# First y tiles written straight into x, products dealt anew over the chunks, and one reciprocal in place of the forward scans

## The reference, cut to what matters

```python
for t in range(S):                       # attention, per batch b and head h
    cur = einsum('bhd,bhe->bhde', u * kt, vt)
    y[:, :, t] = einsum('bhd,bhde->bhe', rt, state + cur)
    state = wt[..., None] * state + einsum('bhd,bhe->bhde', kt, vt)
h = gelu(x @ w_in); u, v = split(h)
v_s = einsum('ts,bsd->btd', w_sg, norm(v) * g_ln) + b_sg
x = x + (u * v_s) @ w_out
u = x + token_mlp(x);  out = u + relu(u @ w_ch1) @ w_ch2
```

## Time and profile before

| what | value |
|---|---|
| median of 3 runs | 410.09 us (410.06 to 410.10) |
| profiled execution | 410.41 us, its span 408.9 us |
| granted TensorE clock, mean | 0.995 |
| busy in the span | TensorE 397.7 us, VectorE 196.7, GpSimd 167.6, ScalarE 109.7 |

### The profile page before, as it was taken

How to read it: one execution, slowest core, us unless ns; L and a number is a source line. 1 busy time by engine, 2 the same in 40 slices (tenths; PEclk the granted TensorE clock), 3 DMA queues, 4 the chain that set the end, 5 groups by cost and what they waited for, 6 DMA issues and landing times.

```text
span 408.9 us, 6916 instructions
## 1 busy us (share of the span) xinstructions
PE 397.7 (97%) x2682; PEld 384.9 (94%) x2682; DVE 196.7 (48%) x402; ACT 109.7 (27%) x218; POOL 167.6 (41%) x186
## 2 busy tenths in 40 slices
PE   6899899999999999999999999999999999999997
PEld 6789788899989999899999999999999999999996
DVE  5688989777977344323442756351132123103301
ACT  3465233464531020475001202340031013002300
POOL 6658659665765355386799990000000000000000
PEclk9999899999999999999999999999999999999999
DMA  9999555473541002002112410000100100000001
GB/s 151 233 202 187 99 117 105 101 145 79 98 135 40 0 2 78 2 1 79 23 55 77 132 63 2 0 2 19 40 0 2 38 21 1 10 31 21 0 21 38
DMA packets 60130, 25.04 MB, mean 61 GB/s; under 512 B 51136, under 2 KB 58176, under 8 KB 60096
## 3 DMA queue, kind: packets, MB, share of 16 engines
q1 hardware_dynamic: 60096, 24.58, 27.0%
HBM read 22.22 MB, written 2.36 MB: 60 GB/s over the span
## 4 chain that ended last, share of the span: by engine, by line
PE 89%; DVE 7%; issue 2%; ACT 1%; DVEq 0%; ACTq 0%
PE bank L1037 24%; PE bank L1039 24%; PE bank L1038 24%; PE bank L1127 4%; PE bank L1051 3%; PE bank L1220 2%; PE bank L1123 2%; PE bank L1160 2%; PE bank L1088 2%; DVE pre L831 1%; DVE suf L822 1%; PE bank L1106 1%; DVE am L855 1%; DVE x L885 1%; PE bank L1178 1%
## 5 line engine op out<-in xcount | busy, mean ns | idle before, releaser
L744 ACT ACTIVATE ha_hi<-bank 128x384 fp32r<-128x384 f32 x48 | 23.6, 492 | 113.1 <-PE bank L1039 113.1
L963 DVE SCALAR_TENSOR_TENSOR ha_lo<-bank,ha_hi 128x384 fp32r<-128x384 f32 x48 | 26.8, 558 | 50.2 <-ACT ha_hi L744 50.2
L1037 PE MATMUL bank<-c_hi,ha_lo 128*128 128x384 f32 x144 | 48.2, 335 | 0.0
L1039 PE MATMUL bank<-c_hi,ha_hi 128*128 128x384 f32 x144 | 48.1, 334 | 0.0
L1039 PE MATMUL bank<-u2T_hi,c_hi 128*128 128x384 f32 x144 | 48.1, 334 | 0.0
L1038 PE MATMUL bank<-c_lo,ha_hi 128*128 128x384 f32 x144 | 48.1, 334 | 0.0
L1037 PE MATMUL bank<-u2T_hi,c_lo 128*128 128x384 f32 x144 | 48.1, 334 | 0.0
L1038 PE MATMUL bank<-u2T_lo,c_hi 128*128 128x384 f32 x144 | 48.1, 334 | 0.0
L968 DVE TENSOR_TENSOR x<-bank,x 128x384 f32<-128x384 f32 x12 | 6.7, 558 | 65.3 <-PE bank L1039 65.3
L1037 PE MATMUL bank<-sg_hi,z_lo 128*128 128x384 f32 x96 | 32.5, 339 | 0.4 <-DVE sg_lo L935 0.4
L1039 PE MATMUL bank<-sg_hi,z_hi 128*128 128x384 f32 x96 | 32.1, 334 | 0.0
(11 more groups left out here) (146 smaller groups left out, 910.7 us busy)
## 6 DMA issues: line engine op xcount, KB each, us to landing
raw<-in_moe_w_ch SPq DMA_DIRECT2D x12, 384.0 KB, 3.1
kc<-in_k SPq DMA_DIRECT2D x12, 192.0 KB, 4.4
rc<-in_r SPq DMA_DIRECT2D x12, 192.0 KB, 4.8
vn<-in_v SPq DMA_DIRECT2D x12, 192.0 KB, 4.4
raw<-in_moe_w_sg SPq DMA_DIRECT2D x6, 384.0 KB, 3.3
out<-x SPq DMA_DIRECT2D x12, 192.0 KB, 1.9
raw<-in_moe_w_in SPq DMA_DIRECT2D x4, 384.0 KB, 4.9
raw<-in_moe_w_tok SPq DMA_DIRECT2D x4, 384.0 KB, 3.3
```

Source lines behind the costliest of these rows:

```text
L744: sc.activation(ha[0][:, i, :], bank[:, 0:HALF], ACT.Relu).then_inc(act_out, 1)
L963: ve.scalar_tensor_tensor(ha[1][:, i, :], bank[:, 0:HALF], 0.0, ha[0][:, i, :].bitcast(F32), ALU.max, ALU.subtract).then_inc(dve_out, 1)
L1037: te.matmul(dst, left[1], right[0], start=first, stop=False)
L1039: return te.matmul(dst, left[0], right[0], start=False, stop=last)
```

## The change

- `decays`: the four forward scans and the 112x4 reciprocal are replaced by one reciprocal of the whole `suf` (112x512), into `pre`. `pre_done` counts 1 per chunk, the semaphore `inverted` is gone, and `turn_w` waits for the suffix scans instead of `pre`.
- `YR` is 5: `y_tile` of chunks 0 to 4 writes straight into x; `x_tile` is left for chunks 5 to 11. The general path overwrites these tiles after waiting for `y_done`. The preset of x leaves out the five tiles. `yt` has three buffers in turn (`BR`), for the diagonal term only.
- `SLOT` begins with chunk 5 in place of 4, the products are dealt anew, and one "sg" product more is in `TAIL`. The w_in splits come one chunk later.
- The ten range checks are in order and spread over chunks 1 to 3; `mark_range`, `sum_range` and `count_range` are in chunk 4.
- SP: v and r before ub, the check tile and k, r, v of later chunks in another order, w one chunk later.
- Filler: 14 matmuls in place of 32, none after chunk 1.

```diff
-YR = 4
+YR = 5
+BR = 3
 SLOT = {
-    (4, 0): [("xT", 0, 0), ("xT", 0, 1)], (4, 2): [("v", 0, 0)],
-    (5, 0): [("v", 0, 1), ("xT", 0, 2)], (5, 1): [("xT", 0, 3)], (5, 2): [("u", 0, 0)],
...
+    (5, 0): [("xT", 0, 0), ("xT", 0, 1)], (5, 1): [("v", 0, 0), ("xT", 0, 2)], (5, 2): [("xT", 0, 3)],
+    (6, 0): [("v", 0, 1), ("xT", 0, 4)], (6, 1): [("v", 0, 2), ("wsg", 0, 0)], (6, 2): [("u", 0, 0), ("wsg", 0, 1)],
+    (7, 0): [("v", 0, 3), ("xT", 0, 5)], (7, 1): [("v", 0, 4), ("wsg", 0, 2)], (7, 2): [("u", 0, 2), ("wsg", 0, 3)],
+    (8, 0): [("v", 0, 5)], (8, 1): [("wsg", 0, 4), ("u", 0, 4), ("wsg", 0, 5)], (8, 2): [("u", 0, 6), ("wsg", 0, 6)],
+    (9, 0): [("wsg", 0, 7), ("u", 0, 1)], (9, 1): [("wsg", 0, 8), ("u", 0, 3), ("wsg", 0, 9)],
+    (9, 2): [("u", 0, 5), ("wsg", 0, 10)],
+    (10, 0): [("wsg", 0, 11), ("u", 0, 7)], (10, 1): [("sg", 0, 0)], (10, 2): [("sg", 0, 1)],
+    (11, 0): [("sg", 0, 2)], (11, 1): [("sg", 0, 3)],
 }
...
                 if n:
                     dve.wait_ge(rp_done, n)
-                ve.reciprocal(pre[0:QP, :, 0:1], suf[0:QP, :, 0:1]).then_inc(inverted, 1)
-                dve.wait_ge(inverted, n + 1)
-                for p in range(NP):
-                    src = bw[0:QP, PART * p:PART * p + PART - 1]
-                    ve.tensor_tensor_scan(pre[0:QP, p, 1:PART], src, ones[0:QP, 1:PART], pre[0:QP, p, 0:1], ALU.mult, ALU.bypass
-                                          ).then_inc(pre_done, 1)
+                ve.reciprocal(pre[0:QP, :, :], suf[0:QP, :, 0:PART]).then_inc(pre_done, 1)
...
-                dst = y_place(n) if n < YR else by[:, 0:C]
-                ve.tensor_tensor(dst, by[:, 0:C], y_place(n), ALU.add).then_inc(y_done, 1)
+                dst = x[:, 0, n, :] if n < YR else by[:, 0:C]
+                ve.tensor_tensor(dst, by[:, 0:C], yt[:, n % BR, :], ALU.add).then_inc(y_done, 1)
...
                 if n == YR - 1:
-                    count_range()
+                    mark_range()
...
                 if n == YR - 1:
-                    bound_x()
-                    x_tile(0)
-                    x_tile(1)
-                if n == YR:
-                    x_tile(2)
-                    x_tile(3)
+                    count_range()
                 y_tile(n)
...
                 if n:
-                    pe.wait_ge(pre_done, NP * n)
+                    pe.wait_ge(suf_done, NP * n)
                 turn(bw, w_tile(n)).then_inc(wt_done, 1)
...
-            keep_busy(4)
+            keep_busy(2)
             turn_w(0)
             turn_k(0)
             turn_r(0)
-            keep_busy(8)
+            keep_busy(2)
             turn_w(1)
+            keep_busy(2)
...
-                if n < YR:
+                if n < 2:
                     keep_busy(2)
                 outputs(n)
...
-                if n < YR:
-                    keep_busy(3)
+                if n < 2:
+                    keep_busy(2)
```

More of the change, by code:

```diff
@@ L60 @@
 SLOT = {
[6 rows of a table removed]
-    (9, 0): [("wsg", 0, 8), ("u", 0, 5)], (9, 1): [("wsg", 0, 9), ("u", 0, 7)], (9, 2): [("wsg", 0, 10), ("wsg", 0, 11)],
-    (10, 0): [("sg", 0, 0)], (10, 1): [("sg", 0, 1)], (10, 2): [("sg", 0, 2)],
-    (11, 0): [("sg", 0, 3)], (11, 1): [("sg", 0, 4)],
[4 rows of a table added]
+    (9, 0): [("wsg", 0, 7), ("u", 0, 1)], (9, 1): [("wsg", 0, 8), ("u", 0, 3), ("wsg", 0, 9)],
[3 rows of a table added]
 }
-TAIL = ([("sg", 0, i) for i in range(5, 8)] + [("xT", 1, i) for i in range(6)] + [("out", 0, i) for i in range(6)]
+TAIL = ([("sg", 0, i) for i in range(4, 8)] + [("xT", 1, i) for i in range(6)] + [("out", 0, i) for i in range(6)]
         + [("v", 1, i) for i in range(6)] + [("u", 1, i) for i in range(8)] + [("sg", 1, i) for i in range(8)]
@@ L175, in build @@
     rku = put("rku", [PART, H, D])
-    yt = put("yt", [PART, YR - 1, C])
+    yt = put("yt", [PART, BR, C])
     ub = put("ub", [PART, C])
@@ L379, in _ @@
             load_k(1)
+            load_r(1)
+            load_v(0)
             sp.dma_start(ub[:, :], u.rearrange("(a h) d -> a (h d)", a=1).to_broadcast([PART, C])).then_inc(ub_in, 16)
-            load_v(0)
-            load_r(1)
             load_w(2)
@@ L394, in _ @@
             load_v(2)
+            load_w(4)
+            load_w(5)
+            sp.dma_start(check_w[:, :].rearrange("p (h x) -> p h x", h=H),
+                         w[1].rearrange("h (p j) d -> p h (j d)", j=PJ)).then_inc(check_in, 16)
+            load_k(4)
+            load_r(4)
+            load_v(3)
             load_raw(0)
             load_raw(1)
-            later = {2: [2], 3: [3, 4], 4: [5], 5: [6], 6: [7], 7: [8], 8: [9, 10], 9: [11], 10: [12], 11: [13, 14]}
-            for n in range(2, NCH):
+            later = {3: [2], 4: [3], 5: [4], 6: [5], 7: [6], 8: [7, 8], 9: [9, 10], 10: [11, 12], 11: [13, 14]}
+            for n in range(3, NCH):
                 if n + 2 < NCH:
@@ L403, in _ @@
                     load_v(n + 1)
-                if NC <= n + 4 < NCH:
-                    load_w(n + 4)
+                if NC <= n + 3 < NCH:
+                    load_w(n + 3)
                 for i in later.get(n, []):
@@ L475, in general_path @@
                 gp.tensor_tensor(gd[:, 1:2], gu[:, 0:1], gu[:, 0:1], ALU.add)
+            pool.wait_ge(y_done, YR)
             for b in range(B):
@@ L502, in _ @@
             for b in range(B):
-                gp.memset(x[:, b, :, :].rearrange("p c n -> p (c n)"), -BIG).then_inc(preset, 1)
+                c = 0 if b else YR
+                gp.memset(x[:, b, c:NC, :].rearrange("p c n -> p (c n)"), -BIG).then_inc(preset, 1)
             gp.memset(wn[:, :, :, D:HP].rearrange("p a h d -> p (a h) d"), 1.0).then_inc(preset, 1)
@@ L509, in split_high @@
                 if name in ("tok1", "tok2"):
-                    pool.wait_ge(x_out, NCH)
+                    pool.wait_ge(x_out, NCH - YR)
                 elif name == "ch1" and i < 4:
@@ L545, in scale_r @@
                 pool.wait_ge(rt_copied, n + 1)
-                pool.wait_ge(pre_done, NP * (n + 1))
+                pool.wait_ge(pre_done, n + 1)
                 if n >= 2:
@@ L554, in diagonal_v @@
                 pool.wait_ge(dg_done, n + 1)
-                if n >= YR:
-                    pool.wait_ge(x_out, n - YR + 2)
-                gp.tensor_tensor(y_place(n).rearrange("p (h d) -> p h d", h=H),
+                if n >= BR:
+                    pool.wait_ge(y_done, n - BR + 1)
+                gp.tensor_tensor(yt[:, n % BR, :].rearrange("p (h d) -> p h d", h=H),
                                  vn[:, n % VR, :].rearrange("p (h d) -> p h d", h=H),
@@ L600, in chunk, with high_part, chunk_end, low_parts @@
                     diagonal_products(n + 1)
-            def chunk_end(n):
+            def high_part(n):
                 if n in early:
                     split_high(*early[n])
+            def chunk_end(n):
+                high_part(n)
                 if n + 1 < NCH:
                     scale_r(n + 1)
+                low_parts(n)
+            def low_parts(n):
                 if n in early:
@@ L619, in rest @@
                 gp.tensor_copy(flag[:, :], nhalf[:, :]).then_inc(flagged, 1)
-                chunk_end(YR - 1)
+                low_parts(YR - 1)
                 for n in range(YR, NCH):
@@ L623, in rest @@
                     chunk_end(n)
-                for i in range(5, 8):
+                for i in range(4, 8):
                     split_gated(0, i)
@@ L649, in _ @@
             chunk(YR - 1)
+            high_part(YR - 1)
+            scale_r(YR)
             pool.wait_ge(ok_counted, 1)
@@ L689, in check_range @@
                 if i:
-                    act.wait_ge(checked, CHECK_ORDER.index(i))
+                    act.wait_ge(checked, i)
                 if i < NC:
@@ L713, in take_job @@
                     elif b and i == 0:
-                        act.wait_ge(x_out, NCH)
+                        act.wait_ge(x_out, NCH - YR)
                     dst = (xT if kind == "xT" else u2T)[b][0]
@@ L774, in _ @@
             check_range(1)
-            checks = {0: (2, 3), 1: (6, 7, 8), 2: (9, 4, 5)}
+            checks = {1: (2, 3), 2: (4, 5, 6), 3: (7, 8, 9)}
             for n in range(NCH):
@@ L883, in x_tile @@
                 dst = x[:, n // NC, n % NC, :]
-                src = y_place(n) if n < YR else by[:, 0:C]
-                ve.scalar_tensor_tensor(dst, src, okm[:, 1:2], dst, ALU.min, ALU.max).then_inc(x_out, 1)
+                ve.scalar_tensor_tensor(dst, by[:, 0:C], okm[:, 1:2], dst, ALU.min, ALU.max).then_inc(x_out, 1)
             def mark_range():
@@ L1011, in _ @@
                     diagonal(n + 1)
+                if n == YR - 1:
+                    bound_x()
                 for b, i in v_jobs(n):
@@ L1113, in outputs @@
                 if n > YR:
-                    pe.wait_ge(x_out, n)
+                    pe.wait_ge(x_out, n - YR)
                 elif n:
@@ L1146, in free_bank @@
                 else:
-                    pe.wait_ge(x_out, NCH)
```

(13 more changed lines are left out.)

21 lines of the change are left out of this document (4 added, 17 removed), and 4 rows, old and new, of the table SLOT.

## The result

| | before | after |
|---|---|---|
| median of 4 runs | 410.10 us (410.06 to 413.89) | 422.82 us (419.94 to 424.51) |
| profiled execution | 410.41 us, span 408.9 | 422.69 us, span 421.2 |
| granted clock, mean | 0.995 | 0.976 |

The change makes the kernel slower, by a ratio of 1.029 (95% interval 1.026 to 1.033). The forecast was 419.6 us.

What follows compares the result with a forecast made beforehand. It took TensorE as the bound, with time won or lost only in chunks 0 to 5. Terms 3.4 + 2.8 + 3.3 gave 9.5 us more: 419.9 us profiled, 419.6 as median; range 410.5 to 431.

Steps and rivals of the forecast that it cites:

- The likeliest case: Whole kernel: the long reciprocal holds up the early chunks, 9.5 us more, 419.6 us; chance 62%.
- The reciprocal is paid per element: VectorE's 112x512 reciprocal: the 24 ns left over recur with every element, 7.0 ns each, so 3.75 us is taken.
- The period 5.3 + R: Chunks 1 to 4: mask to mask takes 5.3 us plus the reciprocal's time R, 9.05 us at full clock.
- The half-way value of the clock: Chunks 1 to 4: period 9.8 us, between full clock and 10.5 at half clock; 39.0 us in place of 36.2.
- Chunk 0 keeps its 6.2 us: Chunk 0 has no decays of its own in its period, so it stays at 6.2 us, from 16.75 to 22.95.
- First mask of chunk 5: Start and chunks 0 to 4: this mask comes at 62.35 us in place of 58.91, 3.4 us later.
- Work not yet done at that mask: Products that stood in chunk 4 now come after chunk 5's first mask: 2.8 us of TensorE work.
- From chunk 5, 3.3 us: Chunk 5 on: TensorE idles 2.2 us in chunk 5, 1.0 in chunk 9, 0.8 elsewhere, less 0.7 idle now.
- three slow x tiles: Chunk 3 before: takes 10.4 us since three x tiles in SBUF take 1.84 us in the mean, not 0.62.
- a reciprocal of 0.7 us: First rival, pipelined reciprocal: first mask 12.3, chunk 5's mask at 46.2, 9.9 us less, 400 us; chance 16%.
- The rest of the change: Chunks 3 and 4 lose 6.7 us of VectorE x tiles, a real gain; other parts such as loads and memset give nothing.

Runs made afterwards that it cites:

- the filler experiment: The kernel after with five filler matmuls added ahead of the state products in chunks 1 to 4: 424.06 us, ratio 1.033.
- two pairs: The kernel after with the reciprocal over two of the four pairs only (112x256), the other forward decays a constant 1: 407.83 us.
- The version in 407.15 us: The kernel after with the four scans back, the old filler in chunks 0 and 1, and three filler matmuls in chunk 4: 407.15 us, ratio 0.9925.

## Why the prediction was right

The likeliest case came about: 422.8 us against 419.6. Point by point:

- **The reciprocal is paid per element.** Right, from a 24 ns remainder: 3.35 us measured, 3.75 taken. That term was too large by 0.4 us, over six places before the mask of chunk 5 some 2.4 us. The row of four elements lies 3 ns over 153 + 4 x 6.25, and 3 ns over four elements become 0.4 us over 512.
- **The period 5.3 + R.** Right: 8.65 and 8.66 us in chunks 1 and 3.
- **The half-way value of the clock, 0.75 us per chunk.** This term was mis-sized: it gave 2.8 us for chunks 1 to 4 (four times 0.75 would be 3.0), and the rows give 0.9. The four chunks take 36.75 us, 1.75 more than 4 x 8.65 and the 0.4 for the range; 0.88 of that is the comparison of 10 elements at 1.04 us in place of 0.16, which the sum had not, and which stood beside GpSimd's work here too. A low clock costs where it covers the scores (chunk 2, 9.41 us), and next to nothing where it lies behind the mask, beside VectorE's reciprocal: chunk 3 takes 8.66 us at a clock of 0.89.
- **Chunk 0 keeps its 6.2 us.** Wrong in the profiled execution: 7.55, since the clock was 0.50 from 20 to 22 us, after an idle of 0.92 us ahead of 17.33. The prediction looked for the low clock in chunks 1 to 4 only. It isn't there in every execution: with the same code up to there, chunk 0 took 6.01 us in the filler experiment.
- **First mask of chunk 5** at 62.35: 60.21. The start and chunks cost 1.3 us, not 3.4.
- **Work not yet done at that mask, 2.8 us.** This term was mis-sized. It counted the products of chunk 4 alone. The timeline before shows that at 58.91 TensorE was through the key transposes of chunk 5 and into the next v product, as VectorE's mask was late; after, the scores end at 60.12, just before the mask. That is about 2.4 us more. TensorE's rows, before and then after:

```profile
56.42 0.60 PE L1095 MATMUL bank<-ident,kp 112*128 112x112 f32 x4
...
57.22 0.48 PE L1037 MATMUL bank<-win_hi,xT_lo 128*128 128x512 f32 x1
```

```profile
58.96 1.16 PE L1086 MATMUL bank<-rp,kp 48*128 48x128 f32 x16 [0.55 <-issue]
60.05 0.85 PE L1093 MATMUL bank<-ident,kp 112*128 112x112 f32 x4
```

- **From chunk 5, 3.3 us.** The idle was sized too large and the clock was left out. Idle in chunks 5, 8, 9 and 10 is 0.77 + 0.24 + 0.76 + 1.31 = 3.1 us, less the 0.7 of before: 2.3. The v product of chunk 5 waits 0.41 us for its copy, not 2.2; the largest idle, in chunk 10, was not foreseen. Chunks 5 and 10 besides ran partly at the low level, about 3.4 us each by their mean clocks of 0.87 and 0.90, half of which is lost, by estimate: 3.4. Together 5.7.

The sum that the rows give is 1.3 + 2.8 + 2.4 + 5.7 = 12.2 us; the spans differ by 12.3. TensorE's busy time supports the middle of it: from the mask of chunk 5 to the end it is 346.4 us before and 355.0 after, 8.6 more, as 2.8 + 2.4 + 3.4. So the total came near by luck in part, as errors offset each other: R and the clock in chunks 1 to 4 too high (2.4 and 1.9 us), the idle behind chunk 5 too high (1.0), against chunk 0 (1.3), the comparison (0.9), the work that TensorE was ahead (2.4) and the clock behind chunk 5 (3.4), which it had at nothing. The sign doesn't hang on them: the reciprocal alone is 14 to 16 us.

Two readings in the prediction are off. Only two of the three slow x tiles stand in chunk 3 (3.26 us from 41.56); the third is in chunk 4. And for a reciprocal of 0.7 us its own terms give a first mask at 10.65, not 12.3; no run shows that case, but with two pairs the mask came later than the terms give (13.59 against 12.75).

The rest of the change was judged right in sign, a gain: the experiment with the reciprocal undone sizes it at 1.6 us. The version in 407.15 us is 3.2 us under the kernel before, but has other filler than the change.

What stays open: which idle is followed by a fall of the clock and which isn't. 0.88 us was in one kernel; 0.87 us (29.23 to 30.10, after) and 1.2 us (14.34 to 15.54, before) were not. Executions of one kernel differ too: 407.0 us at 1.000, 408.6 at 0.995, 411.4 at 0.988 in the best version.

## What to carry to other kernels

Before one long instruction takes the place of several short ones, look for the same operation in the trace at another size and divide what it takes over the base of a one-element instruction by its elements: here 28 ns over 4 elements told 3.7 us for 512, and 3.35 were measured: each ns of error in the short row is 0.13 us in the long one, so bound the value from both sides. Then see what is queued behind it on its engine; the cost multiplies with each place at which the loop waits for that engine. And compare two kernels at the same event only after asking how far each engine is ahead there.

## What the runs showed of the hardware that was not expected

- A VectorE reciprocal costs 6.25 ns per element (1753, 2553 and 3353 ns for 256, 384 and 512), a running product by scan about 1.95 ns, by estimate from its 402 ns for 128 elements and the same base ((402 - 153) / 128).
- A VectorE comparison of 10 elements took 0.16 us before, 1.04 after and 2.41 with the range marked earlier; the two long ones ended together with an instruction of GpSimd.
- What the granted clock is worth in the best version: 407.0 us at a mean of 1.000, 408.6 at 0.995 and 411.4 at 0.988. Idles of TensorE as short as 0.88 and 1.31 us came before falls to 0.50.
